# When three transitions of an attention and two-MoE kernel are re-ordered: weight chunks sent earlier, a copy ahead of the gates' parts, an id map ahead of two waits

## The chip, the cores and the metric

One core of a Trainium2 chip. The metric is the device time of one execution in microseconds (us), the median of several runs. Lower is better.

## The reference

Three stages, one after the other. B, H, S, D = 2, 8, 768, 64; the 1536 tokens have 512 columns.

```
# 1. causal attention with a decay for each head
state = gamma * state + k_t v_t^T;   y_t = scale * q_t state
x = y laid out as [1536 tokens, 512]
# 2. first MoE, 8 experts, F = 1024, top-1, with a residual
do = (x @ w_skip) > 0;  e = argmax(x @ w_gate);  g = softmax(x @ w_gate)[e]
x[do] += g * (relu(x @ w1[e]) @ w2[e])
# 3. second MoE, 8 experts, top-1, each expert takes its first `capacity` tokens in order
out = g2 * (relu(x @ v1[e]) @ v2[e])   for kept tokens, else 0
```

## The kernel before, in words

The kernel is written engine by engine, with semaphores between the engines: SyncE (SP) issues nearly all loads, GpSimd (POOL) the indirect gathers and scatters, ScalarE (ACT) copies out of PSUM and rounds, VectorE (DVE) does the routing arithmetic and the low halves of split numbers, TensorE (PE) the matmuls. Each engine runs its own list in order; a wait holds all that stands behind it on that engine.

**Attention** has 16 steps (STEPS), two batches of eight (four head pairs, two halves of the sequence). In each step PE makes scores, updates, outputs (`o_done` counts them) and turns the result into token rows, which ACT stores to the DRAM tensor `x_rows` (`store_rows`). SP loads the second batch's inputs in the first eight steps. From loop index n = FIRST_WEIGHTS on, SP then sends one chunk of expert weights for each index, `first_chunk(k)`, after it has waited for `o_done` to reach n. A chunk is a quarter of one expert: 1 MB, two chunks of w1 and two of w2. `raw` holds eight of them: slots 0 to 3 for the even expert of a pair, 4 to 7 for the odd one. Before, FIRST_WEIGHTS is 9 and WEIGHTS_DURING is 6, so chunks 0 to 5 go out in attention and chunks 6 and 7 (the w2 half of expert 1) later: SP first sends `w_wide` (the next router's weights, broadcast to all partitions, after ACT has written `w_next`), then waits for the gather of expert 1's rows, `gathered[0][1]`, and only then sends the last two. Behind them in SP's list stands `load_pair`, which sends a chunk for a later expert whenever `chunk_used[c]` says that its slot is free.

**Routing before the first MoE.** The rows of the first nine groups of tokens (EARLY) are ranked and stored during attention; of the last three the rows are still in SBUF. The first job's rows are put together from both: PE's `turn_early` multiplies the late rows by a 0/1 matrix (`spread`) and adds the early rows (`y_t`, an indirect gather issued by POOL after `early_ids`) by four transposes. The two halves of the result go from PSUM to `x_f`, one by ACT (`copy_first`), one by DVE (`copy_half`, which signals `x_half_done`); PE's first hidden layer waits for both. PE meanwhile maps tokens to slots (`map_ids`, into `ps_e`), DVE turns that into `slot_id` (`ids_ready`), and POOL gathers rows for experts 1, 0, 2 and 3. The gate values are split into three bf16 parts by `gate_parts` and multiplied out to `carried_g`; PE maps these too (line 1642), between its two hidden chunks, and DVE sums the result into `slot_gate`.

**A layer** is a loop over windows (one is needed here) and in it over eight jobs, one for each expert, software-pipelined by `step`: output of this job, turn of the next job's rows, hidden layer of the next. The first MoE uses the raw f32 weights for the hidden layer; for the output, and for both in the second MoE, a weight is split in a rounded high part (`w_hi`, ACT, line 768) and a low part (`w_lo`, DVE, line 1102) and each product is three matmuls. In the first MoE DVE also scales and adds (`add_y`) and makes the next router's logits (`next_logits`). A job of the first MoE has 128 slots, one of the second 256.

**Between the MoEs** the last job's rows are turned and routed on chip: `late_logits`, `choose_late`, `late_counts`; PE adds the late rows to the first rows of the second MoE (line 1667, after `late_placed`), maps slots (`map_next`) and counts (`cross_counts`, which signals `slots_mapped[1]`). The last step of the window is a map of the next block of slots, `map_ids(range(G), ps_y[:, 1, :], early_mapped)`: DVE waits for it in `find_early`, and POOL then gathers the rows of a further window, should there be one. The second MoE begins with POOL's two gathers of the first rows (`gather_first`, `first_in`), PE's `turn_first`, then `copy_first` on ACT and `copy_half` on DVE. On DVE, `split(first, 0)` and the waiting for `slots_mapped[1]` stand ahead of that `copy_half`:

```
if i == 1:
    split(first, 0)
...
else:
    hold(dve, slots_mapped[1], w + first_maps)
```

`keep_clock` is a matmul of zeros that nothing reads.

Of the kernel before, what the change touches and what calls it, by code (L numbers as in the profile page):

```python
# [6 lines left out]
ALU = mybir.AluOpType  # L7
# [11 lines left out]
E, F = 8, 1024  # L19
KD = DM // P  # L20
G = N // P
CH = S // P
HP = H // 2
HC = CH // 2
FIRST_WEIGHTS = 9
WEIGHTS_DURING = 6
STEPS = B * 2 * HP
# [3 lines left out]
NV = 5  # L31
NID = 2
# [38 lines left out]
def repeat(x, dim, n):  # L71

    y = x.unsqueeze(dim)
    return y.broadcast_to([*y.shape[:dim], n, *y.shape[dim + 1:]])
# [31 lines left out]
def program(nc, q_cols, k_cols, k_rows, v_rows, w_route, moe_w1, moe_w2, moe2_w1, moe2_w2, capacity, consts, out):  # L106
# [8 lines left out]
    with ExitStack() as ctx:  # L115
# [304 lines left out]
        def _(sp):  # L420
# [47 lines left out]
            def first_chunk(k):  # L468

                load_chunk(LAYERS[0], Job(LAYERS[0], 0, 0, 0, k // 4), k % 4)  # L470
# [14 lines left out]
            for k in range(2):  # L485
                sp.wait_ge(rows_stored[k], 48)
            sp.dma_start(w_wide[:].rearrange("p e d -> p (e d)"), w_next.rearrange("e d -> (e d)").partition_broadcast(P)
                         ).then_inc(w_wide_in, 16)
            sp.wait_ge(gathered[0][1], 16)
            for k in range(WEIGHTS_DURING, 8):  # L490
                first_chunk(k)

# [185 lines left out]
        def _(act):  # L678
# [71 lines left out]

            for part in range(2):
                if part == 1:
                    exp_part(1)
                store_extra(part)
            act.wait_ge(w_turn, 1)
            nc.scalar.copy(w_turned[:], ps_y[0:E, 0, :]).then_inc(w_copied, 1)
            act.wait_ge(w_copied, 1)
            act.dma_start(w_next, w_turned[:]).then_inc(w_stored, 16)

            base = 0  # L760
# [110 lines left out]
        def _(dve):  # L871
# [225 lines left out]
            for layer in LAYERS:  # L1097
# [123 lines left out]
                with dve.Fori(0, win.reg) as w:  # L1221
# [5 lines left out]
                    if i == 0:  # L1227
                        for a in range(2):
                            hold(dve, next_free[a], w * (E // 2) * 16 + 16)
                        dve.wait_ge(exp_done[0], 2)  # L1230
                        gates(EARLY, G, wchain)
                        gate_parts(vals, G, wchain)
                        nc.vector.tensor_tensor(carried_g[:], repeat(vals[:, :, NID:], 3, E), repeat(hot_b[:], 2, NV - NID),
                                                ALU.mult).then_inc(gates_carried[0], 1)
                        copy_half(first)
# [6 lines left out]
                    nc.vector.tensor_tensor(ids, found_id[:, 0:tb], found[:, :, 1], ALU.add).then_inc(ids_ready[i], 1)  # L1242
                    if i == 0:
                        count_windows(0, wchain)
                        split(first, 2)
# [60 lines left out]
        def _(pe):  # L1306
# [154 lines left out]
            for layer in LAYERS:  # L1461
# [162 lines left out]
                with pe.Fori(0, win.reg) as w:  # L1624
# [25 lines left out]
                    if i == 0:  # L1650
# [12 lines left out]
                        late_counts(1)  # L1663
                        keep_clock(ps_h[:, 0, :], 1)
                        pe.wait_ge(late_placed, w + 1)
# [6 lines left out]
                        cross_counts().then_inc(slots_mapped[1], 1)  # L1672
                        hold(pe, slots_ready[0], w + 2)
                        map_ids(range(G), ps_y[:, 1, :], early_mapped)
                    else:
# [38 lines left out]
```

## Time and profile before

| | us |
|---|---|
| median of 3 runs | 394.72 (393.82 to 396.45) |
| the profiled execution, its time | 392.57 |
| the profiled execution, its span | 390.5 |
| PE busy in the span | 377.3 |

The span is from the first to the last instruction; 2.07 us of the profiled execution lie around it. The median of the runs is 2.15 us above the profiled execution. In the trace attention lasts to about 72 us, the first MoE from there to about 185, the second from about 193 to the end. A row of the timeline gives the start, the duration, the engine, the line, the operation with its tiles, and in brackets how long the engine stood idle before it and what ended that.

### The profile page before, as it was taken

To read this page: it belongs to the slowest core of one execution; us is meant where nothing else is said; L and a number is where in the kernel's file an instruction comes from. 1 tells how busy PE (TensorE), PEld (TensorE's weight loads), DVE (VectorE), ACT (ScalarE), POOL (GpSimd) and SP (SyncE) were. 2 spreads that over 40 slices of the span, in tenths; PEclk is the share of its full clock that TensorE was granted. 3 is DMA by queue.
4 is the path that set the end of the run, shared out by engine and by line. 5 is a ranking of instruction groups with operands and counts; after the bars stand their busy time and mean duration, and the time that the engine had idled before them with its cause. 6 is when DMAs were issued, how large, how long until landed. Compare 5 with 4: busy or idle time off the path is not lost.

```text
span 390.5 us, 7690 instructions
## 1 busy us (share of the span) xinstructions
PE 377.3 (97%) x2870; PEld 339.1 (87%) x2870; DVE 263.9 (68%) x479; ACT 170.2 (44%) x216; POOL 90.1 (23%) x89
## 2 busy tenths in 40 slices
PE   8999999799899999999889999999999999999996
PEld 5888887799799989998678998989989898998983
DVE  2876878789999889878497757364574636558340
ACT  2454453424434542450544356455453744445410
POOL 5010000181444232330524021402104040130103
PEclk9999999999999999999999999999999999999999
DMA  7999998489999999719497999666748566540102
GB/s 261 365 379 384 350 349 278 123 309 384 390 389 388 389 390 385 277 24 392 121 360 249 339 388 334 210 223 223 238 165 282 201 212 233 168 151 0 54 0 89
DMA packets 56179, 101.97 MB, mean 261 GB/s; under 512 B 6751, under 2 KB 18527, under 8 KB 56017
## 3 DMA queue, kind: packets, MB, share of 16 engines
q1 hardware_dynamic: 46048, 85.67, 61.6%
q0 software_dynamic: 4736, 12.13, 9.2%
q10 hardware_dynamic: 5360, 3.70, 3.1%
q8 instruction: 23, 0.38, 0.4%
q14 instruction: 12, 0.09, 0.1%
HBM read 90.44 MB, written 12.73 MB: 264 GB/s over the span
## 4 chain that ended last, share of the span: by engine, by line
PE 85%; DMA 6%; issue 3%; DVE 2%; SPq 1%; ACT 1%; POOL 0%; DVEq 0%; ACTq 0%; POOLq 0%
PE ps_h L1532 35%; PE ps_y L1560 30%; PE ps_r L1376 3%; PE ps_o L1357 3%; PE ps_s L1322 3%; PE ps_y L1576 3%; PE ps_u L1336 3%; DMA raw<-in_moe_w 3%; PE ps_t L1468 2%; PE ps_o L1349 2%; DMA k_in<-in_k_rows 2%; DMA xg<-x_rows,slot_id 1%; PE ps_t L1667 1%; PE ps_t L1599 1%; ACT w_hi L768 0%
## 5 line engine op out<-in xcount | busy, mean ns | idle before, releaser
L1102 DVE TENSOR_TENSOR w_lo<-raw,w_hi 128x2048 fp32r<-128x2048 f32 x48 | 109.2, 2288 | 20.2 <-ACT w_hi L768 19.7
L768 ACT CAST w_hi<-raw 128x2048 fp32r<-128x2048 f32 x48 | 90.5, 1904 | 7.7 <-DMA raw<-in_moe_w 5.5
L1120 DVE SCALAR_TENSOR_TENSOR h_lo<-ps_h,h_hi 128x512 fp32r<-128x512 f32 x48 | 33.1, 690 | 57.8 <-ACT h_hi L785 57.6
L1560 PE MATMUL ps_y<-w_hi,h_hi 128*128 128x512 f32 x176 | 70.7, 402 | 1.4 <-DVE h_lo L1120 1.4
L1560 PE MATMUL ps_y<-w_hi,h_lo 128*128 128x512 f32 x176 | 68.8, 391 | 0.0
L1560 PE MATMUL ps_y<-w_lo,h_hi 128*128 128x512 f32 x176 | 68.7, 390 | 0.0
L785 ACT ACTIVATE h_hi<-ps_h 128x512 fp32r<-128x512 f32 x48 | 28.7, 598 | 90.6 <-PE ps_h L1532 90.6
L1532 PE MATMUL ps_h<-x_f,raw 128*128 128x128 f32 x512 | 59.2, 275 | 1.1 <-DVE x_f L1113 1.1
L1532 PEld LDWEIGHTS ps_h<-x_f,raw 128*128 128x128 f32 x512 | 58.5, 192 | 1.7 <-issue 1.2
L1532 PE MATMUL ps_h<-x_hi,w_hi 128*128 128x256 f32 x256 | 41.1, 283 | 1.9 <-DVE x_hi L1113 1.9
L556 POOL DMA_INDIRECT xg<-x_rows,slot_in x14 | 15.2, 1087 | 114.9 <-ACT yo L796 105.2
L1532 PE MATMUL ps_h<-x_hi,w_lo 128*128 128x256 f32 x256 | 41.0, 283 | 0.0
L1532 PE MATMUL ps_h<-x_lo,w_hi 128*128 128x256 f32 x256 | 41.0, 283 | 0.0
L1560 PEld LDWEIGHTS ps_y<-w_hi,h_hi 128*128 128x128 f32 x176 | 33.1, 188 | 7.5 <-ACT h_hi L785 1.5
L1560 PEld LDWEIGHTS ps_y<-w_hi,h_lo 128*128 128x128 f32 x176 | 33.0, 188 | 7.2
L1560 PEld LDWEIGHTS ps_y<-w_lo,h_hi 128*128 128x128 f32 x176 | 33.2, 188 | 5.9
L1532 PEld LDWEIGHTS ps_h<-x_hi,w_hi 128*128 128x128 f32 x256 | 35.6, 191 | 2.8 <-issue 2.2
L1532 PEld LDWEIGHTS ps_h<-x_lo,w_hi 128*128 128x128 f32 x256 | 35.3, 192 | 0.0
L1532 PEld LDWEIGHTS ps_h<-x_hi,w_lo 128*128 128x128 f32 x256 | 35.2, 192 | 0.0
L1144 DVE SCALAR_TENSOR_TENSOR product<-yo,w_wide 128x512 f32<-128x512 f32 x48 | 30.3, 688 | 0.0
L581 POOL DMA_INDIRECT out<-yo,slot_out x16 | 16.0, 1002 | 39.1 <-ACT yo L796 20.9
L556 POOL DMA_INDIRECT xg<-x_rows,slot_id x8 | 17.8, 2221 | 25.3 <-DVE yo L1132 16.5
(198 smaller groups left out, 430.0 us busy)
## 6 DMA issues: line engine op xcount, KB each, us to landing
raw<-in_moe_w SPq DMA_DIRECT2D x64, 1024.0 KB, 8.2
q_t<-in_q_cols SPq DMA_DIRECT2D x16, 192.0 KB, 4.8
k_t<-in_k_cols SPq DMA_DIRECT2D x16, 192.0 KB, 6.2
k_in<-in_k_rows SPq DMA_DIRECT2D x15, 192.0 KB, 6.4
v_in<-in_v_rows SPq DMA_DIRECT2D x15, 192.0 KB, 6.4
out<-zero SPq DMA_DIRECT2D x1, 2816.0 KB, 10.7
w_wide<-w_next SPq DMA_DIRECT2D x1, 2048.0 KB, 7.0
x_rows<-rows ACTq DMA_DIRECT2D x4, 384.0 KB, 6.7
```

The lines of the kernel that those rows point to most:

```text
L556: nc.gpsimd.indirect_dma_start(out=job.rows_of(t), out_offset=None, in_=x, in_offset=bass.IndirectOffsetOnAxis(ap=ids[t], axis=0), bounds_ ...
L581: nc.gpsimd.indirect_dma_start(out=target, out_offset=bass.IndirectOffsetOnAxis(ap=rows_at, axis=0), in_=yo[:, job.par, t * DM:(t + 1) * D ...
L768: nc.scalar.copy(w_hi[c], raw[:, 4 * job.par + c, :]).then_inc(hi_done[c], 1)
L785: nc.scalar.activation(h_hi[:, g * 512:(g + 1) * 512], ps_h[:, g % 2, :], ACT.Relu).then_inc(h_hi_done[i], 1)
L1102: nc.vector.tensor_tensor(w_lo[c], raw[:, 4 * job.par + c, :], w_hi[c].bitcast(F32), ALU.subtract).then_inc(lo_done[c], 1)
L1120: nc.vector.scalar_tensor_tensor(out=h_lo[:, cols], in0=ps_h[:, g % 2, :], scalar=0.0, in1=h_hi[:, cols].bitcast(F32), op0=ALU.max, op1=AL ...
L1144: last = nc.vector.scalar_tensor_tensor(out=product[:, e], in0=yo[:, job.par, 0:DM], scalar=1.0, in1=w_wide[:, e], op0=ALU.mult, op1=ALU.m ...
L1322: last = pe.matmul(ps_s[:, p, a, c * P:(c + 1) * P], k_t[part, hp, toks], q_t[part, hp, toks], start=True, stop=True)
L1336: last = pe.matmul(ps_u[:, c * P:(c + 1) * P], k_dec[:, p, c].rearrange("p a d -> p (a d)"), v_in[:, hp, half * HC + c].rearrange("p a d - ...
L1357: last = pe.matmul(ps_o[a * D:(a + 1) * D, c * P:(c + 1) * P], v_in[:, hp, c0 + c, a, :], probs[:, p, a, c, :], start=False, stop=True, sk ...
L1532: last = pe.matmul(dst, wt[:, kk * QF + fb * P:kk * QF + (fb + 1) * P], xt[:, kk, :], start=(kk == 0 and z == 0 and not (first and g == 0 ...
L1560: last = pe.matmul(ps_y[:, t, :], ht, wt, start=(fb == 0 and z == 0), stop=(fb == 2 * QB - 1 and z == 2))
```

## The change

Three places are touched. The numbers of chunks and their place in SP's list: FIRST_WEIGHTS 8 and WEIGHTS_DURING 8, so that all eight chunks are sent in the attention loop, and the wait for `gathered[0][1]` with the two chunks behind it goes. ACT's list after attention: the copy of the turned router weights and its store to `w_next` come first, then the second `exp_part`, then both `store_extra`. DVE's list at the start of the first MoE: `gate_parts` and `carried_g` move behind `copy_half` and the slot ids. PE's list at the end of the first MoE: `map_ids` of the next block of slots moves ahead of the wait for `late_placed`, in the place of one `keep_clock`.

```
-FIRST_WEIGHTS = 9
-WEIGHTS_DURING = 6
+FIRST_WEIGHTS = 8
+WEIGHTS_DURING = 8
...
-            sp.wait_ge(gathered[0][1], 16)
-            for k in range(WEIGHTS_DURING, 8):
-                first_chunk(k)
...
-            for part in range(2):
-                if part == 1:
-                    exp_part(1)
-                store_extra(part)
             act.wait_ge(w_turn, 1)
             nc.scalar.copy(w_turned[:], ps_y[0:E, 0, :]).then_inc(w_copied, 1)
             act.wait_ge(w_copied, 1)
             act.dma_start(w_next, w_turned[:]).then_inc(w_stored, 16)
+            exp_part(1)
+            for part in range(2):
+                store_extra(part)
...
                         gates(EARLY, G, wchain)
-                        gate_parts(vals, G, wchain)
-                        nc.vector.tensor_tensor(carried_g[:], repeat(vals[:, :, NID:], 3, E), repeat(hot_b[:], 2, NV - NID),
-                                                ALU.mult).then_inc(gates_carried[0], 1)
                         copy_half(first)
                         dve.wait_ge(slots_mapped[0], w + 1)
...
                     nc.vector.tensor_tensor(ids, found_id[:, 0:tb], found[:, :, 1], ALU.add).then_inc(ids_ready[i], 1)
                     if i == 0:
+                        gate_parts(vals, G, wchain)
+                        nc.vector.tensor_tensor(carried_g[:], repeat(vals[:, :, NID:], 3, E), repeat(hot_b[:], 2, NV - NID),
+                                                ALU.mult).then_inc(gates_carried[0], 1)
                         count_windows(0, wchain)
                         split(first, 2)
...
                         late_counts(1)
-                        keep_clock(ps_h[:, 0, :], 1)
+                        hold(pe, slots_ready[0], w + 2)
+                        map_ids(range(G), ps_y[:, 1, :], early_mapped)
                         pe.wait_ge(late_placed, w + 1)
...
                         cross_counts().then_inc(slots_mapped[1], 1)
-                        hold(pe, slots_ready[0], w + 2)
-                        map_ids(range(G), ps_y[:, 1, :], early_mapped)
```

## Rows read from the trace of the kernel before

**Rows 1.** The page, busy time of each engine.

```profile
PE 377.3 (97%) x2870; PEld 339.1 (87%) x2870; DVE 263.9 (68%) x479; ACT 170.2 (44%) x216; POOL 90.1 (23%) x89
```

**Rows 2.** Windows; busy time of each engine (instructions), clock, DMA share, GB/s.

```profile
66.00:68.00 2.00, 2.00 (x29) 1.67 (x28) 1.31 (x7) 0.77 (x3) 0.00 (x0) 1.00 0.35 127
68.00:70.00 2.00, 1.74 (x18) 1.59 (x15) 0.99 (x7) 0.47 (x3) 0.43 (x1) 1.00 0.09 30
81.00:95.30 14.30, 14.30 (x104) 13.23 (x104) 13.95 (x34) 4.56 (x5) 5.43 (x6) 1.00 0.93 325
100.00:180.00 80.00, 80.00 (x578) 73.78 (x577) 69.20 (x138) 33.19 (x32) 26.28 (x16) 1.00 0.90 330
198.00:384.50 186.50, 186.50 (x1260) 170.57 (x1259) 107.53 (x109) 88.13 (x84) 34.27 (x33) 1.00 0.60 208
```

**Rows 3.** Chain that ended last, 55 to 100 us: start, duration, what.

```profile
77.85 5.66 DMA xg<-x_rows,slot_id
...
83.94 10.13 DMA raw<-in_moe_w
```

**Rows 4.** Timeline, all engines, 92 to 100 us: start, duration, instruction, idle before.

```profile
94.09 1.90 ACT L768 CAST w_hi<-raw 128x2048 fp32r<-128x2048 f32 x1 [3.12 <-DMA raw<-in_moe_w]
...
96.03 2.29 DVE L1102 TENSOR_TENSOR w_lo<-raw,w_hi 128x2048 fp32r<-128x2048 f32 x1 [0.68 <-ACT w_hi L768]
96.20 3.00 POOL L556 DMA_INDIRECT xg<-x_rows,slot_id  x1 [9.17 <-DVE yo L1132]
...
99.07 0.47 PE L1560 MATMUL ps_y<-w_hi,h_hi 128*128 128x512 f32 x1 [1.37 <-DVE h_lo L1120]
```

**Rows 5.** Timeline, all engines, 69 to 86 us.

```profile
69.57 1.09 POOL L614 DMA_INDIRECT y_t<-x_rows,early_id  x1 [40.45 <-DMA x_rows<-slots]
...
72.62 0.57 ACT L756 COPY w_turned<-ps_y 8x512 f32<-8x512 f32 x1 [0.95 <-issue]
...
74.81 0.60 PE L1496 MATMUL ps_t<-iw,y_t 128*128 128x128 f32 x4
74.96 0.19 DVE L989 CAST vals<-gate 128x12 bf16<-128x12 f32 x1
...
75.81 0.34 SPq L487 DMA_DIRECT2D w_wide<-w_next  x1
76.13 0.42 DVE L1113 COPY x_f<-ps_t 128x256 f32<-128x256 f32 x1
...
76.80 3.83 PE L1532 MATMUL ps_h<-x_f,raw 128*128 128x128 f32 x32 [1.10 <-DVE x_f L1113]
...
80.95 0.17 DVE L1248 COPY gate_sum<-ps_e 128x8 f32<-128x8 f32 x1 [1.21 <-PE ps_e L1642]
```

**Rows 6.** DMA issues of 69 to 71 us: instruction, count, us to landing.

```profile
y_t<-x_rows,early_id POOLq DMA_INDIRECT x1, 3.6
```

**Rows 7.** DMA issues of 58.5 to 62 us.

```profile
raw<-in_moe_w SPq DMA_DIRECT2D x1, 1024.0 KB, 7.9
```

**Rows 8.** Timeline, all engines, 188 to 198 us.

```profile
189.11 0.68 PE L1310 MATMUL ps_h<-zero 128*128 128x256 f32 x2
...
189.97 1.99 PE L1667 MATMUL ps_t<-late_hot,yo 128*128 128x256 f32 x8 [0.17 <-DVE late_hot L1289]
...
192.45 0.45 PE L1434 MATMUL ps_y<-carried,slots 128*128 128x16 bf16 x12
193.04 0.16 DVE L1056 TENSOR_SCALAR early_found<-ps_y 128x1 f32<-128x1 f32 x1 [2.93 <-PE ps_y L1434]
...
193.57 1.06 PE L1476 MATMUL ps_t<-iw,xg 128*128 128x128 f32 x8 [0.68 <-DMA xg<-x_rows,first_id]
...
193.87 2.29 DVE L1102 TENSOR_TENSOR w_lo<-raw,w_hi 128x2048 fp32r<-128x2048 f32 x1 [0.48 <-issue]
...
196.37 0.68 DVE L1113 CAST x_hi<-ps_t 128x512 fp32r<-128x512 f32 x1
...
197.35 1.18 PE L1532 MATMUL ps_h<-x_hi,w_hi 128*128 128x256 f32 x8 [1.85 <-DVE x_hi L1113]
```

## The prediction

> **What bounds the kernel now.** I first read the busy time of each engine on the page: PE is at work in 97% of the span [rows 1]. Then I asked for windows to see where the missing 3% lie. From 100 to 180 us PE is busy 80.00 of 80.00 us, and from 198 to 384.5 us 186.50 of 186.50 [rows 2]. The reader should take two things from this. Nothing that this change does for DMA, DVE or ACT in these two stretches can win time there. And whatever is won ahead of 100 or ahead of 198 us is handed on whole to the end, since PE's own list paces all that follows. So only two stretches matter: 70 to 100 us (attention to first MoE) and 185 to 198 us (first to second MoE).
>
> In the first, PE's last idle time is 1.37 us at 99.07, put down to DVE's h_lo [rows 4]. The chain that ended last shows where this comes from: the gather of expert 1's rows, 5.66 us from 77.85, then, since SP waits for it, weight chunk 7, sent at 83.94 and landed 10.13 us later, at 94.07 [rows 3]. ACT stood 3.12 us idle for this chunk and DVE 0.68 us for ACT [rows 4]. The other idle time is 1.10 us at 76.80, where the first hidden layer waits for DVE's half of x_f [rows 5]. In the second stretch PE waits 1.85 us at 197.35 for the same kind of copy by DVE [rows 8].
>
> **The copy ahead of the gates' parts.** Before, DVE ran gate_parts and carried_g from 74.96 to 76.13, 1.17 us, and then copy_half, 0.42 us. Its input was complete when PE's four transposes ended, 74.81 + 0.60 = 75.41 [rows 5]. Now DVE has finished the gates by 74.96 and waits; with 0.1 us for the signal it copies from 75.5 to 75.92, in place of 76.13 to 76.55. PE started 0.25 us after the copy, at 76.80; now at 76.17. That is 0.63 us on the path. ACT's half was never the later one: it needs only the first two transposes. What is moved is not free on DVE: 1.17 us of work now lies behind the slot ids, ahead of the window count and of the w_lo of chunk 2. The cover is the idle time before gate_sum: 1.21 us [rows 5]. DVE's list got there at 79.74; now at 79.74 - 0.63 + 1.17 = 80.28. PE's map of the gates is ready at 80.95 - 0.63 = 80.32. So the cover is just used up, and DVE goes on 0.6 us earlier than before. The same map on PE needs carried_g, done by about 77.4, 3 us before PE comes to it. The slot ids, and POOL's first gather with them, come some 0.45 us earlier (the copy is no longer behind the 1.17 us, but the ids now follow it at once).
>
> **All chunks in attention.** SP's loop waits for o_done 8 at n = 7 as well as at n = 8, so chunk 0 now goes out right behind the last inputs of the second batch; chunks 1 to 6 at the moments when 0 to 5 went, and chunk 7 one step later, about 64.4 us (the last one went at 60.75). The inputs of the second batch are all in the queue ahead of chunk 0, so attention itself doesn't see it. The two chunks must then find room. A chunk at 330 GB/s for 0.90 of the engines [rows 2] is 1.05 MB / 367 GB/s = 2.9 us of transfer, two are 5.7. The engines are free for 0.65 of 66 to 68 and 0.91 of 68 to 70 us [rows 2], 3.1 us. Chunk 5 landed 7.9 us after its issue [rows 7], at 68.7. So chunk 7 lands at about 72, at the latest at 68.7 + 5.7 = 74.4 us. Both are long ahead of the time when ACT first wants chunks 6 and 7, some 88 us for the one and 94.09 less 3.12 for the other [rows 4]. What comes to lie beside it is the early gather (69.57, landed after 3.6 us, 73.2 [rows 5, 6]); PE needs it at 74.81, so it has 1.6 us of cover. I take its delay as at most 1 us, no cost, and keep the other end for the slower rival.
>
> At the other end, ACT can convert chunk 3 of expert 1 (raw slot 7) as soon as PE has used up the same part of expert 0. PE was free for the output at 99.07 - 1.37 = 97.70 and the hidden layer before it has 64 matmuls; 32 took 3.83 us [rows 5], so the chunk was free at 90.0 or little later. ACT is through by 92.5 in place of 95.99. Now DVE is the later one. It was busy 13.95 of 14.30 us from 81.00 to 95.30 [rows 2], so it keeps its 0.63 us and no more until there; then its 0.68 us of idle time goes. The w_lo starts at 96.03 - 0.63 - 0.68 = 94.72, and PE's output at 99.07 - 1.31 = 97.76. PE is ready at 97.70 - 0.63 = 97.07, so 0.69 us of its wait stay, with DVE's own list as the cause. **Gain of the first stretch: 1.31 us.**
>
> SP loses its wait for the gather, and behind that wait stood load_pair. Its first chunk, for expert 2, can now go at about 80.5, when the first hidden chunk is used. It shares the engines with the gathers for experts 1, 0, 2 and 3. PE turns expert 1's rows at about 86.6; the gather took 5.66 us beside the 2 MB of w_wide [rows 3]. Issued at 77.4, it may take 9 us before it costs anything. I take nothing.
>
> **ACT's new order.** The router weights' copy starts at 70.9 in place of 72.62 [rows 5], so w_next and w_wide (before at 75.81) go 1.7 us earlier. The exp comes 0.6 us later, about 72.1, and DVE wants it past 74. The two small stores go last, one us later; POOL asks for them only behind four gathers. Worth nothing, cost nothing: next_logits first reads w_wide behind the h_lo for which PE waits at 99.07.
>
> **The map of the next block moved.** Before, it was PE's last item, 0.45 us at 192.45; DVE had come to it at 193.04 - 2.93 = 190.11 and waited. Only then did DVE leave the loop and start the first w_lo of the second MoE at 193.87 for 2.29 us, then the slot ids, and copy_half at 196.37 to 197.05; PE began 0.30 us later [rows 8]. Now the map takes the slot of one keep_clock at 189.11 (0.68 us), so the eight matmuls at 189.97, which wait for late_hot, aren't held up. DVE passes find_early at 190.1, starts the w_lo 0.83 us later, at 190.95, and is done at 193.24; the slot ids by 193.6 (cross_counts stands ahead of the map at 192.45 in PE's list, so it is through by then). What is late next is the first rows: PE's turn_first started at 193.57 on the DMA of the gather and took 1.06 us, to 194.63 [rows 8]. POOL's list ahead of that gather isn't touched, so this stays. DVE's copy then runs from 194.7 to 195.38, PE begins at 195.68. **Gain of the second stretch: 197.35 - 195.68 = 1.67 us.** POOL's gather for the further window goes out some 1.6 us earlier; it stands behind the first rows' gathers in POOL's list. The dummy matmuls that are dropped cost 0.68 us in which PE waited anyway. The granted clock is 1.00 in all the windows I read [rows 2], 2.4 GHz, through gaps longer than the 0.3 us by which the one before turn_first grows.
>
> **Two rules of the Trainium skill.** While DVE made w_lo from 96.03, POOL's issue of a gather took 3.00 us, where it took 1.09 us at 69.57 [rows 4, 5]: it was held until DVE was done, and DVE's duration didn't change. The Trainium skill ("SBUF — State Buffer", Who interferes with whom) says that the one who issues first holds the shared ports and the other blocks. By the page the gather, at 77.4, would now be ahead of the w_lo, at 78.1, and hold DVE until 78.5, and the first stretch would give about 0.9 us. The trace shows only the other order, so the page stands beside the rival of a smaller gain. The same section infers that tensor_tensor leaves the writing of descriptors alone; the row at 96.20 says otherwise.
>
> **Rivals.** (1) DVE's cover, 80.28 against 80.32, is a tie. If DVE comes 0.4 us late there, or the 1.17 us isn't covered, DVE is the bound through to 99 us and the first stretch gives between 0 and 0.9 us: 394.72 - 1.67 - 0.4 = 392.7. For it: DVE is at 98% from 81 to 95 us. (2) The second stretch gives nothing, because PE or DVE is held there by something that lay under the old wait: 394.72 - 1.31 = 393.4. Against it: DVE's whole chain is in the rows. (3) The waits that I leave in place shrink too, 0.69 us at the output and 0.68 us for the first rows [rows 8]: 391.74 - 1.37 = 390.4. (4) **Slower:** chunks 6 and 7 keep the queues full and the early gather is late. It costs from the point at which it lands after 74.81, and outweighs the gains after 77.8. If it took as long as chunk 7 did in the full queues, 10.13 us [rows 3], it would land at 79.7 and PE's transposes would come 4.9 us later: 391.74 + 4.9 = 396.6. For it: the engines still have about 2 us of chunk to move at 70 us. Against it: the gather has only 0.25 MB, and the one at 77.85 landed in 5.66 us beside w_wide. The Trainium skill ("DMA: Bandwidth & Descriptors", Queues, rings and completion order) says that an engine takes its queues in turn, packet by packet; by that rule the gather doesn't stand behind the chunk.
>
> **How the numbers follow.** Forecast: 1.31 + 1.67 = 2.98 us. The profiled execution would go from a span of 390.5 to 387.5 and from 392.57 to 389.6; from the median, 2.15 us above that execution, 394.72 - 2.98 = 391.7. Chances: forecast 0.52, (1) 0.17, (2) 0.06, (3) 0.15, (4) 0.05, and 0.05 for a gather that is late by 1 to 3 us and eats most of the gain, about 394. The range reaches from just under (3), 390.2, to 395.0, and leaves out most of (4). A difference of 1%, 3.9 us, is about what a measurement of this kernel can tell from no change; the forecast lies within it. Faster by more would need (3) or a median half a microsecond off: 0.18. Slower by more needs (4) at its full price and more: 0.03.
>
> **What the profile would show.** Right: the first hidden matmul at about 76.2; chunks 6 and 7 landed by 74; no ACT wait for raw before 95; the first output of expert 1 at about 97.8 with 0.7 us of idle time; from there on everything 1.3 us earlier, find_early right behind DVE's last place; turn_first and the hidden layer of the second MoE 2.1 us apart. Wrong: idle PE before the transposes of turn_early or before the first turn (DMA), a w_lo of DVE longer than 2.3 us (ports), a granted clock below 1.00 near 190 us, or new idle PE inside 100 to 180 us.

## The result and the profile after

Four executions of each kernel, side by side: 394.34 us before, 389.25 us after (388.70 to 389.89). The ratio is 0.9861, 95% interval 0.982 to 0.9903: 1.4% faster, 5.1 us. The forecast was 391.7, within 390.2 to 395.0; the time is 1 us below the range. The profiled execution went from 392.57 to 389.74, by 2.83 us, which is nearly the forecast's 2.98. So in sum the change did to the profiled execution what was worked out, and to the median 1.7 times as much. Where the other 2 us come from is the main question below.

That the profiled execution meets the forecast so closely is in part luck. Four rows cut the time in pieces, the 24 matmuls with spread (`turn_early`) and the 26 of `map_next`, before and then after:

```profile
72.03 2.94 PE L1492 MATMUL ps_t<-spread,slots 128*128 128x128 f32 x24 [0.40 <-DVE spread L1089]
...
185.17 0.81 PE L1418 MATMUL ps_e<-carried,slots 128*128 128x16 bf16 x26
```

```profile
71.55 2.94 PE L1488 MATMUL ps_t<-spread,slots 128*128 128x128 f32 x24 [0.40 <-DVE spread L1085]
...
183.09 0.81 PE L1414 MATMUL ps_e<-carried,slots 128*128 128x16 bf16 x26
```

From spread to expert 1's output it is 25.46 us in place of 27.04, so 1.58 us less, forecast 1.31. From map_next to the second MoE's hidden layer it is 11.55 us in place of 12.18, so 0.63 us less, forecast 1.67. The 0.48 us by which attention ended earlier in this execution fills most of the gap, and is not the change's doing: spread began between 71.33 and 72.25 us in the traces of all the kernels, in no order of the edits.

In the code after, the same instructions stand three or four lines higher (L1532 is L1528, L1560 is L1556, L1310 is L1306). The page after, span and busy time:

```profile
span 387.8 us, 7686 instructions
...
PE 376.2 (97%) x2868; PEld 338.6 (87%) x2868; DVE 263.6 (68%) x479; ACT 170.4 (44%) x216; POOL 89.0 (23%) x89
```

Windows of the changed kernel, with the columns of [rows 2]. PE is again without a gap from 100 to 180 and from 198 on. The two added chunks are seen in the DMA share of 66 to 70 us, 1.06 and 0.66 where it was 0.35 and 0.09:

```profile
66.00:68.00 2.00, 1.74 (x26) 1.32 (x26) 1.09 (x7) 1.23 (x4) 0.00 (x0) 1.00 1.06 382
68.00:70.00 2.00, 1.92 (x16) 1.55 (x16) 1.14 (x8) 0.48 (x1) 0.90 (x1) 1.00 0.66 255
...
100.00:180.00 80.00, 80.00 (x578) 73.65 (x577) 69.04 (x139) 33.51 (x32) 25.89 (x16) 1.00 0.87 306
...
198.00:381.00 183.00, 183.00 (x1234) 167.22 (x1234) 104.87 (x105) 88.02 (x84) 35.29 (x33) 1.00 0.62 210
```

The early gather and chunk 7 in the changed kernel, us to landing (before 3.6, and 7.9 for the last chunk [rows 6, 7]). Chunk 7 was sent at 64.0 and was there at 70.8. The gather took 0.2 us more of its 1.6 us of cover, but 3.8 us is also what it took in before_again, copy_only and map_only, which don't have chunk 7 beside it:

```profile
y_t<-x_rows,early_id POOLq DMA_INDIRECT x1, 3.8
```

```profile
raw<-in_moe_w SPq DMA_DIRECT2D x1, 1024.0 KB, 6.8
```

Timeline of the changed kernel after attention, to be read beside [rows 5]. The copy on DVE starts 0.04 us after the four transposes end (74.33 + 0.60), and the hidden layer 1.31 us after they began, where it was 1.99: 0.68 us, forecast 0.63. w_lo ends at 77.49 + 2.28 = 79.77 and gate_sum follows at 79.80, without idle time. That is the tie of the forecast, 80.28 against 80.32, less the 0.48 us by which attention ended earlier in this execution (the transposes at 74.33 in place of 74.81); DVE lost nothing by it:

```profile
74.07 0.34 SPq L487 DMA_DIRECT2D w_wide<-w_next  x1
...
74.33 0.60 PE L1492 MATMUL ps_t<-iw,y_t 128*128 128x128 f32 x4
...
74.97 0.42 DVE L1109 COPY x_f<-ps_t 128x256 f32<-128x256 f32 x1 [0.52 <-PE ps_t L1492]
...
75.64 3.83 PE L1528 MATMUL ps_h<-x_f,raw 128*128 128x128 f32 x32 [0.42 <-DVE x_f L1109]
...
76.70 1.03 POOL L553 DMA_INDIRECT xg<-x_rows,slot_id  x1 [6.50 <-issue]
...
77.49 2.28 DVE L1098 TENSOR_TENSOR w_lo<-raw,w_hi 128x2048 fp32r<-128x2048 f32 x1
...
79.80 0.17 DVE L1244 COPY gate_sum<-ps_e 128x8 f32<-128x8 f32 x1
...
80.92 2.35 DVE L1098 TENSOR_TENSOR w_lo<-raw,w_hi 128x2048 fp32r<-128x2048 f32 x1
80.94 0.99 POOL L553 DMA_INDIRECT xg<-x_rows,slot_id  x1 [0.30 <-issue]
```

Expert 1 in the changed kernel, beside [rows 4]. ACT no longer waits for DMA; the second conversion waits 0.43 us for PE, as the chunk's slot must be used up. PE's output begins at 97.01 after 0.48 us of waiting, put down to DVE:

```profile
87.14 1.91 ACT L764 CAST w_hi<-raw 128x2048 fp32r<-128x2048 f32 x1
...
89.48 1.90 ACT L764 CAST w_hi<-raw 128x2048 fp32r<-128x2048 f32 x1 [0.43 <-PE ps_y L1556]
...
93.98 2.29 DVE L1098 TENSOR_TENSOR w_lo<-raw,w_hi 128x2048 fp32r<-128x2048 f32 x1
...
97.01 0.47 PE L1556 MATMUL ps_y<-w_hi,h_hi 128*128 128x512 f32 x1 [0.48 <-DVE h_lo L1116]
```

The second transition, beside [rows 8]. The map is at 187.18 in the place of the dummy, find_early at 187.95, the first w_lo at 188.77; from turn_first to the hidden layer it is 2.09 us, where it was 3.78. But turn_first waits 2.04 us for the rows, where it waited 0.68:

```profile
187.18 0.45 PE L1430 MATMUL ps_y<-carried,slots 128*128 128x16 bf16 x12
...
187.95 0.15 DVE L1052 TENSOR_SCALAR early_found<-ps_y 128x1 f32<-128x1 f32 x1
...
188.77 2.29 DVE L1098 TENSOR_TENSOR w_lo<-raw,w_hi 128x2048 fp32r<-128x2048 f32 x1 [0.48 <-issue]
...
192.55 1.07 PE L1472 MATMUL ps_t<-iw,xg 128*128 128x128 f32 x8 [2.04 <-DMA xg<-x_rows,first_id]
...
193.66 0.69 DVE L1109 CAST x_hi<-ps_t 128x512 fp32r<-128x512 f32 x1 [2.31 <-PE ps_t L1472]
...
194.64 1.19 PE L1528 MATMUL ps_h<-x_hi,w_hi 128*128 128x256 f32 x8 [0.16 <-issue]
```

### The profile page after: what moved, and what is told of

It reads as the page before. It is cut to its first block, busy times and chain, and to the rows that moved or that the text cites. A ratio compares the mean times of both kernels' runs of the same rounds, so it can differ in the third digit from the quotient of the medians.

```text
span 387.8 us, 7686 instructions
## 1 busy us (share of the span) xinstructions
PE 376.2 (97%) x2868; PEld 338.6 (87%) x2868; DVE 263.6 (68%) x479; ACT 170.4 (44%) x216; POOL 89.0 (23%) x89
## 3 DMA queue, kind: packets, MB, share of 16 engines
HBM read 90.44 MB, written 12.73 MB: 266 GB/s over the span
## 4 chain that ended last, share of the span: by engine, by line
PE 89%; DMA 3%; issue 2%; DVE 2%; SPq 1%; ACT 1%; POOL 0%; ACTq 0%; POOLq 0%; DVEq 0%
PE ps_h L1528 37%; PE ps_y L1556 31%; PE ps_o L1353 3%; PE ps_s L1318 3%; PE ps_r L1372 3%; PE ps_y L1572 3%; PE ps_u L1332 3%; PE ps_t L1464 2%; PE ps_o L1345 2%; DMA xg<-x_rows,first_id 1%; DMA k_in<-in_k_rows 1%; PE ps_t L1488 1%; DVE above L1255 0%; SPq L442 0%; SPq L430 0%
## 5 line engine op out<-in xcount | busy, mean ns | idle before, releaser
L1556 PE MATMUL ps_y<-w_hi,h_hi 128*128 128x512 f32 x176 | 70.7, 402 | 0.5 <-DVE h_lo L1116 0.5
L1556 PE MATMUL ps_y<-w_hi,h_lo 128*128 128x512 f32 x176 | 68.7, 391 | 0.0
L1556 PE MATMUL ps_y<-w_lo,h_hi 128*128 128x512 f32 x176 | 68.7, 390 | 0.0
L1528 PE MATMUL ps_h<-x_f,raw 128*128 128x128 f32 x512 | 59.2, 275 | 0.4 <-DVE x_f L1109 0.4
L1528 PEld LDWEIGHTS ps_h<-x_f,raw 128*128 128x128 f32 x512 | 58.5, 192 | 1.1 <-issue 0.5
L553 POOL DMA_INDIRECT xg<-x_rows,slot_in x14 | 16.5, 1177 | 114.8 <-ACT yo L792 105.3
L1528 PE MATMUL ps_h<-x_hi,w_hi 128*128 128x256 f32 x256 | 41.1, 283 | 0.2 <-issue 0.2
L1528 PE MATMUL ps_h<-x_hi,w_lo 128*128 128x256 f32 x256 | 41.0, 283 | 0.0
L1528 PE MATMUL ps_h<-x_lo,w_hi 128*128 128x256 f32 x256 | 41.0, 283 | 0.0
L1556 PEld LDWEIGHTS ps_y<-w_hi,h_lo 128*128 128x128 f32 x176 | 33.0, 188 | 7.1
L1556 PEld LDWEIGHTS ps_y<-w_hi,h_hi 128*128 128x128 f32 x176 | 33.1, 188 | 6.6 <-issue 0.6
L1556 PEld LDWEIGHTS ps_y<-w_lo,h_hi 128*128 128x128 f32 x176 | 33.2, 188 | 5.9
L1528 PEld LDWEIGHTS ps_h<-x_hi,w_hi 128*128 128x128 f32 x256 | 35.6, 191 | 1.1 <-issue 0.5
L1528 PEld LDWEIGHTS ps_h<-x_lo,w_hi 128*128 128x128 f32 x256 | 35.3, 192 | 0.0
L1528 PEld LDWEIGHTS ps_h<-x_hi,w_lo 128*128 128x128 f32 x256 | 35.2, 192 | 0.0
L553 POOL DMA_INDIRECT xg<-x_rows,slot_id x8 | 15.5, 1932 | 26.0 <-DVE yo L1128 17.9
```

Source lines behind the costliest of these rows:

```text
L553: nc.gpsimd.indirect_dma_start(out=job.rows_of(t), out_offset=None, in_=x, in_offset=bass.IndirectOffsetOnAxis(ap=ids[t], axis=0), bounds_ ...
L1528: last = pe.matmul(dst, wt[:, kk * QF + fb * P:kk * QF + (fb + 1) * P], xt[:, kk, :], start=(kk == 0 and z == 0 and not (first and g == 0 ...
L1556: last = pe.matmul(ps_y[:, t, :], ht, wt, start=(fb == 0 and z == 0), stop=(fb == 2 * QB - 1 and z == 2))
```

## The experiments

All were timed in turns with the kernel before, in three series. Over the three the kernel before ran 80 times (two further executions, at 424 and 752 us, are left out as disturbed). The list of executions gives the span and the mean granted clock of each, and this turned out to be the key. before_again, chunks_only, copy_only and map_only are of the first series, after_again, before_fill, after_fill and after_no_chunks of the second, the rest of the third. The kernel before had 391.2, 391.7 and 390.9 us at full clock in the three, so spans of different series compare to about half a microsecond only:

| kernel | executions | median us | of these at clock 0.998 or more | their median span | spans of the rest |
|---|---|---|---|---|---|
| before | 80 | 394.94 | 17 | 391.2 | 391.7 to 396.5 |
| after | 10 | 389.52 | 8 | 387.4 | 387.9, 388.1 |
| chunks_only | 12 | 393.04 | 5 | 389.7 | 390.9 to 391.7 |
| copy_only | 12 | 396.24 | 2 | 391.85 | 392.3 to 395.9 |
| map_only | 12 | 392.65 | 3 | 388.5 | 389.9 to 393.5 |
| before_fill | 12 | 393.83 | 10 | 391.8 | 391.3, 392.5 |
| after_fill | 6 | 390.87 | 6 | 389.0 | |
| after_no_chunks | 10 | 392.06 | 4 | 389.35 | 389.5 to 392.9 |
| after_no_map | 9 | 391.11 | 6 | 389.0 | 389.9 to 390.3 |
| chunks_map | 6 | 389.48 | 6 | 387.45 | |
| after_turn | 6 | 388.56 | 4 | 386.4 | 387.9, 388.5 |
| after_plus | 6 | 387.95 | 4 | 385.55 | 386.9, 387.2 |

**before_again**: the kernel before, unchanged.

> The kernel before, unchanged, profiled and timed once more. Theory A (the gain beyond my sum comes from a chain through DMA that is longer in most executions than in the one profiled): its span is 391.5 to 394 us, and the chain from the slot ids over the gather for expert 1 to the landing of chunk 7 (94.07 - 76.82 = 17.2 us in the first trace) is longer by the same 1 to 3 us; PE's first output of expert 1 comes after 99.07. Theory B (the two medians of few runs are simply off by some microseconds): ratio to the kernel before 0.997 to 1.003 here, and the span and PE's first output again within 0.5 us of 390.5 and 99.07. Theory C (attention differs): the time of PE's first hidden matmul (76.80) moves by over 1 us.

394.65 us, ratio 1.0007 (0.9975 to 1.0039); the profiled span is 393.2 at a mean clock of 0.996. Attention is the same: the first hidden layer starts at 76.89 (76.80). Two things differ from the first trace. The chain through DMA is longer, 6.67 us for the gather and 10.11 for chunk 7, which is issued and lands 1.1 us later:

```profile
77.96 6.67 DMA xg<-x_rows,slot_id
...
85.06 10.11 DMA raw<-in_moe_w
```

and PE's wait, in the list of waits, is 2.4 us in place of 1.4:

```profile
PE ps_y L1560 <- DVE h_lo L1120: 2.4, 1, 2.4
```

Then, after PE had stood still from 98 to 100 us, the granted clock fell to about half, the 1.2 GHz level (windows; the clock is the number ahead of the DMA share). In these four microseconds PE issued 11 matmuls, and in the next two, at full clock, 13:

```profile
98.00:100.00 2.00, 0.00 (x0) 0.00 (x0) 2.00 (x3) 0.43 (x1) 1.70 (x2) 1.00 1.05 387
100.00:102.00 2.00, 1.84 (x5) 1.54 (x6) 2.00 (x8) 0.00 (x0) 0.32 (x1) 0.62 1.05 390
102.00:104.00 2.00, 2.00 (x6) 1.52 (x6) 2.00 (x6) 0.00 (x0) 0.00 (x0) 0.53 1.04 387
```

From the output to map_next this execution needed 87.69 us; the first trace had 86.10. So one such stretch costs 1.6 us. The other traces bear this out: from the output to map_next all without a fall there need 86.08 to 86.21 us, and after_no_chunks, which has one, 87.58 (copy_only, with a longer one, 88.83). The first trace had clock 1.00 throughout; only 17 of 80 executions have a mean of 0.998 or more. Theory A holds for 1 us. Theory B has the ratio for it and the span and the output against it. The clock was in no theory yet.

**chunks_only**: only the chunks moved.

```
-FIRST_WEIGHTS = 9
-WEIGHTS_DURING = 6
+FIRST_WEIGHTS = 8
+WEIGHTS_DURING = 8
...
-            sp.wait_ge(gathered[0][1], 16)
-            for k in range(WEIGHTS_DURING, 8):
-                first_chunk(k)
```

> Only the chunks moved into attention, nothing else. My sum of the prediction: the wait at 99.07 shrinks by DVE's 0.68 us only, so 0.7 us less. Theory A: 2 to 3.5 us less in the median, since this part alone takes the gather and the chunk off the chain. Theory B: 0.7 us, as in the sum.

Ratio 0.993 (0.9905 to 0.9954), 1.9 us less in the median; between executions at full clock 1.5 us (391.2 to 389.7). PE's wait at expert 1's output was 0.6 us. The clock now falls in 7 of 12 executions, at most once: in the profiled one behind 196 us, at the second transition, and not behind 99.

**copy_only**: gate_parts and carried_g behind the slot ids.

> Only gate_parts and carried_g moved behind the slot ids. The slot ids come 0.45 us earlier, and with them the gather and chunk 7: the chain through DMA is 0.45 us shorter, so 0.45 us less at 99.07; by the sum 0.63 us is the most it can give. Theory A and B agree here: 0.4 to 0.7 us.

Both theories missed: ratio 1.0021 (0.9992 to 1.0049), no gain. The slot ids came earlier, and so the gather went out together with w_wide, which SP sends at its old time:

```profile
76.47 0.34 SPq L487 DMA_DIRECT2D w_wide<-w_next  x1
```

The chain shows the gather beside it: 8.30 us, where it was 5.66 [rows 3]. It was issued 1.4 us earlier than in the first trace and let SP send chunks 6 and 7 from 84.80 on, 1.3 us later than there (83.53). The chain now runs over chunk 6, the row at 84.80, for which ACT stood 4.8 us idle:

```profile
76.48 8.30 DMA xg<-x_rows,slot_id
...
84.80 7.04 DMA raw<-in_moe_w
```

```profile
PE ps_y L1560 <- DVE h_lo L1120: 3.4, 1, 3.4
```

PE waited 3.4 us, of which 0.7 us because it was ready earlier, and the clock fell for longer, from 98 to 106 us (windows):

```profile
98.00:100.00 2.00, 0.31 (x1) 0.34 (x2) 2.00 (x3) 0.00 (x0) 1.82 (x1) 0.68 1.04 386
...
102.00:104.00 2.00, 2.00 (x6) 1.61 (x5) 2.00 (x6) 0.00 (x0) 0.00 (x0) 0.50 1.05 389
```

Ten of twelve executions had a low clock. Here an earlier gather was no gain, since it gated two chunks and met w_wide. ACT's new order, which sends w_wide earlier, is not in this run, and no run has it by itself.

**map_only**: map_ids of the next block ahead of the wait for late_placed.

> Only map_ids of the next block moved ahead of the wait for late_placed. My sum: 1.67 us less. If the landing of the first rows moves later with it, as the trace of the changed kernel hints (turn_first 0.96 us later against PE's arrival than before), 0.6 to 0.9 us less. Rival: this part is worth more than 2.5 us in the medians, which would put the missing 2 us here and not in DMA ahead of the first MoE.

Ratio 0.9952 (0.9919 to 0.9984), 2.3 us in the median, 2.7 between the few at full clock (388.5, three executions). The rows landed 4.3 us after the later gather was issued, where it was 4.7; the fear of a later landing isn't borne out here. The expectation of 1.67 us is exceeded by 1 us at full clock. In the profiled execution the clock was low right at this transition (windows), and the eight matmuls with late_hot took 3.49 us in place of 1.99; before it PE had only short matmuls with waits between them:

```profile
190.00:192.00 2.00, 1.74 (x18) 1.41 (x17) 1.42 (x8) 1.89 (x2) 1.54 (x2) 0.77 0.63 188
192.00:194.00 2.00, 2.00 (x6) 1.38 (x5) 1.93 (x1) 0.00 (x0) 1.84 (x1) 0.50 0.48 166
194.00:196.00 2.00, 1.94 (x36) 1.84 (x35) 0.35 (x2) 0.30 (x1) 1.70 (x2) 0.87 0.24 52
```

At expert 1's output, on the other hand, PE waited 2.2 us in this execution, after the same 1.1 us at 76.8 as in before_again, and the clock didn't fall:

```profile
98.00:100.00 2.00, 0.16 (x1) 0.19 (x2) 2.00 (x3) 0.32 (x1) 2.00 (x1) 1.00 1.04 386
100.00:102.00 2.00, 2.00 (x10) 1.61 (x9) 2.00 (x7) 0.00 (x0) 0.00 (x0) 1.00 1.04 387
```

**after_again**: the changed kernel once more.

> The changed kernel again, to count its granted clocks. Theory D (clock): the four parts win their microseconds on the path, and on top of that the kernel before loses 1.6 us in each of the 1 to 2 stretches of some 3.4 us at 1.2 GHz that 35 of its 46 executions show behind the two transitions; the changed kernel has few of them. So: nearly all executions at a mean clock of 0.998 or more, median near 389, and a spread of spans under 2 us. Theory E (the gain is on the path alone, the clock is the same for both): two executions in three show 0.996 or 0.991 again and the median is 390 to 391.

389.53 us; five of six executions at clock 1.000, spans 387.1 to 388.1, while 17 of 20 of the kernel before beside them were below 0.997. Theory D stands, Theory E falls: the change takes away most of the falls.

**before_fill**: the kernel before with dummy matmuls in PE's waits.

```
+                    if i == 0 and this.e == 1:
+                        keep_clock(ps_y[:, 1, :], 3)
                     output(this, 2)
...
-                        pe.wait_ge(x_half_done, w + 1)
                         pe.wait_ge(w_copied, 1)
+                        keep_clock(ps_h[:, 0, :], 2)
+                        pe.wait_ge(x_half_done, w + 1)
...
                         turn_first(first)
-                        keep_clock(ps_h[:, 0, :], 2)
+                        keep_clock(ps_h[:, 0, :], 6)
```

> The kernel before with matmuls of zeros put where PE waits (2 ahead of the wait for x_half_done, 3 ahead of expert 1's output, 4 more behind turn_first); nothing on the path is shortened. Theory D: fewer executions with a low clock, median 1 to 2 us below before, the executions at clock 1.000 near 391.2 us of span as before or a little above. Theory E: no gain, or slower by the few tenths that a filler delays the path.

Nothing on the path is shorter, and the executions at full clock are 0.6 us longer (391.8) than the 391.2 of all series; in the trace map_next to the hidden layer is 12.73 us in place of 12.18. Yet the median fell to 393.83 against 395.43 beside it (the same series), ratio 0.9965 (0.994 to 0.999), and ten of twelve executions kept the clock. Its profile has 1.00 in both windows where the others fell:

```profile
98.00:104.00 6.00, 6.00 (x31) 5.04 (x31) 6.00 (x18) 1.86 (x3) 2.77 (x2) 1.00 1.05 387
196.00:202.00 6.00, 4.86 (x37) 4.44 (x36) 5.75 (x9) 1.19 (x4) 1.83 (x1) 1.00 1.06 398
```

The profiled execution is one of the two with a low mean, 0.996: its clock fell ahead of all the added matmuls, in attention's last microseconds (72 to 74 us at 0.50), and the 24 matmuls with spread took 4.13 us. That cost nothing that shows, as expert 1's output still came at 99.16, where it was 99.07: there PE has to wait for DVE's h_lo anyway.

```profile
70.00:72.00 2.00, 1.52 (x8) 0.70 (x8) 1.64 (x10) 0.41 (x2) 0.39 (x1) 0.71 0.40 72
72.00:74.00 2.00, 2.00 (x10) 2.00 (x11) 1.34 (x8) 0.57 (x1) 0.00 (x0) 0.50 0.94 227
```

This run shows the clock as a cause by itself: 1.6 us of median, by the interval 0.4 to 2.4 us, with 0.6 us of path paid for it.

**after_fill**: fillers of 1, 1 and 4 in the changed kernel, the last ahead of turn_first.

> The changed kernel with fillers of the same kind (1, 1, and 4 in the 2 us wait ahead of turn_first). Theory D: at most a few tenths below the changed kernel, since few low-clock stretches are left to remove; 388.5 to 389.5. Theory E: same as the changed kernel or 0.3 us slower.

390.87 us, slower than the changed kernel. The clock was full in all six, as it nearly was without. The four fillers stood in PE's list until 193.8 and the rows had been there since 192.4 (SP, which waits for the same rows, sent its next chunk at 192.47): a filler in a wait of unknown length becomes the wait.

**after_no_chunks**: the changed kernel with six chunks in attention and two behind the gather.

> The changed kernel with only six chunks in attention, the last two behind the gather again. By the clean executions (chunks alone: span 391.2 to 389.7, 1.5 us) the stall at expert 1's output comes back at 1.4 to 3.4 us and the clean span is 388.2 to 388.5. Theory D: this stall also brings back the low clock behind it in over half of the executions, so the median is 2.5 to 4 us above the changed kernel's. Theory E: 1.5 us above.

392.06 us, 2.5 above the changed kernel; at full clock 389.35, 1.95 above (1.75 above the 387.6 of the same series); six of ten with a low clock. The chain through DMA is back, 5.71 and 11.40 us, and PE waits 2.7 us:

```profile
77.36 5.71 DMA xg<-x_rows,slot_id
...
83.50 11.40 DMA raw<-in_moe_w
```

```profile
PE ps_y L1559 <- DVE h_lo L1119: 2.7, 1, 2.7
```

**after_no_map**: the changed kernel with the map at PE's end.

> The changed kernel with the map of the next block back at PE's end. Clean spans (mean clock of 0.998 or more) against the changed kernel's 386.7 to 388.0: by the traces the map is worth 0.6 to 1.5 us at the second transition, so 388.3 to 389.3. Clock theory D: PE's 1.9 us of waiting behind turn_first is back, and with it 1.2 GHz stretches behind 195 us in a good part of the executions, as in 7 of 12 with the chunks alone; median 390.5 to 391.5. Without a part for the clock: 390.1 to 390.8.

391.11 us; at full clock 389.0 against 387.4, so the map is worth 1.6 us beside the other parts, forecast 1.67. Three of nine had a low clock, too few to move the median beyond these 1.6 us.

**chunks_map**: chunks and map, without the copy and ACT's order.

> The kernel before with the chunks and the map moved, without the copy and ACT's order. It tells what the copy and ACT's order add: by the prediction 0.63 us on the path, so a clean span of 387.4 + 0.6 = 388.0 and a median of 390.0. If the copy is worth nothing in company either, as it was alone, 389.5 and the clock as for the changed kernel. If its 1.1 us of waiting at the first hidden layer brings the low clock back, 391.

389.48 us, 387.45 at full clock: the same as the changed kernel. In the traces the copy does show at expert 1's output, 25.46 and 25.59 us behind the first matmul with spread in place of 26.26. It isn't in the time: at the second transition, map_next to the hidden layer, this kernel needed 10.01 us, the changed one 10.67 and 11.55, since its later gather of first rows landed later.

The pair chunks_only and after_no_map differs by the copy and ACT's order too, and there they are in the time. The output comes 25.46 us behind spread in place of 26.27, the two stretches behind it are the same (86.13 and 86.10 us, then 12.18 and 12.19), and the executions at full clock have 389.0 us in place of 389.7; they are of different series, in which the kernel before had 390.9 and 391.2.

**after_turn**: a semaphore for each gather of first rows, and turn_first by blocks.

```
-                    hold(pe, first_in, (n_first + w) * 32)
-                    for kk in range(KD):
-                        for t in range(tb):
+                    for t in range(tb):
+                        hold(pe, (first_in0, first_in)[t], (n_first + w) * 16)
+                        for kk in range(KD):
```

> The changed kernel, and turn_first takes each block of first rows as it lands (a semaphore for each gather), so that 4 and not 8 transposes stand behind the later gather. The wait for that gather is what the second transition ends on: half of 1.06 us less, so 0.5 us below the changed kernel. If the wait lay elsewhere, no change.

388.56 us, and at full clock 386.4 against 387.4, twice what was expected. In the trace map_next to the hidden layer takes 9.59 us. chunks_map, in whose trace the later gather took the same 4.2 us to land, needed 10.01. So 0.4 us are the new order of the transposes; the rest can't be told from an earlier landing than in the changed kernel's two traces.

**after_plus**: the same, and the two halves of above moved behind the logits of experts 2 and 4.

```
-                        for j in range(LATE):
-                            last = nc.vector.tensor_tensor(above[:, j], ...)
-                        last.then_inc(above_ready, 1)
...
                         next_logits(this, range(E // 2, E))
+                        if this.e in (2, 4):
+                            j = this.e // 2 - 1
+                            last = nc.vector.tensor_tensor(above[:, j], ...)
+                            if j == LATE - 1:
+                                last.then_inc(above_ready, 1)
```

> The same, and DVE's two comparisons for above (1.71 us each) are moved from the first job behind the logits of experts 2 and 4. The 0.5 us for which PE still waits at expert 1's output is DVE's list, so it goes: another 0.5 us less, 1.0 us below the changed kernel. Rival: the two pieces don't fit beside the later jobs, where DVE has about 1.1 us to spare before PE wants h_lo, and PE waits there instead; then no gain or up to 1 us lost against the previous one.

387.95 us, ratio to the kernel before 0.9823 (0.9783 to 0.9863); 385.55 at full clock, 0.85 below after_turn. The wait at the output is gone from PE's list of waits, and no other took its place. What is left of the longest waits around the first MoE is the last o_t of attention and the first hidden layer:

```profile
PE ps_o L1350 <- ACT o_t L695: 0.5, 1, 0.5
...
PE ps_h L1533 <- DVE x_f L1112: 0.4, 1, 0.4
```

It is the fastest of all. Against the changed kernel it wins 1.6 us by medians of six and ten executions, from different series; two of the six still had a low clock, the profiled one from 186 to 192 us.

## Why the prediction was right or wrong

**Wrong: the clock.** The step that failed reads: "The granted clock is 1.00 in all the windows I read [rows 2], 2.4 GHz, through gaps longer than the 0.3 us by which the one before turn_first grows." It is true of the profiled execution and false of the kernel, and the step built on it, "from the median, 2.15 us above that execution, 394.72 - 2.98 = 391.7", carries the 2.15 us over as if the change couldn't touch them. 63 of 80 executions had a mean clock below 0.998, in the traces that caught one by falls to 1.2 GHz at one or both transitions, at 1.5 to 1.6 us a time, and the median of all is 1.75 us of span above those at full clock (392.95 against 391.2). The changed kernel kept its clock in 8 of 10, and its median of all is only 0.25 us above those at full clock (387.65 against 387.4). So about 1.75 of the 2.15 us were the clock, and the change took away 1.5 of them. The profiled execution, 390.5 us of span, was moreover shorter than any of the 17 at full clock. The sign of it stood in the figures: it took 392.57 us and the lowest of the three timed ones 393.82. Without this part the time would have lain in the range, at about 390.9.

What makes the clock fall in one execution and not in the next is not shown. Fewer and shorter waits of PE went with fewer falls: 63 of 80 before, 7 of 12 with the chunks alone, 9 of 12 with the map alone, 2 of 16 with both (the changed kernel and chunks_map). But after_turn and after_plus, whose waits are shorter still, have 4 of 12, and in after_plus's trace the fall is where the waits are 0.2 and 0.3 us (186 to 192 us). What before_fill shows is that filling the waits of the kernel before takes most of its falls away.

**Wrong: the size of the chunks' term.** I had 0.68 us, DVE's idle time in the one trace. Measured: 1.5 us alone and 1.95 us in company, at full clock. The stall was set by two transfers in a row, and the first trace had the shortest draw of five with this chain: PE waited 1.4 us there, 2.4 in before_again and 2.2 in map_only, and 3.4 in copy_only and 2.7 in after_no_chunks, of which 0.7 us are PE's being ready earlier. That DVE's list would be what is left was right: 0.48 us of wait, forecast 0.69, and after_plus removed it by moving DVE's work.

**Right in mechanism, luck in the number: the map.** From turn_first to the hidden layer it is 2.09 us in place of 3.78, 1.69 less, forecast 1.67. Rival (2) falls. "What is late next is the first rows" was right too, but "so this stays" was not: they can land earlier or later. So the map's worth at full clock is 1.6 us beside all the others (after_no_map), 2.25 beside the chunks (chunks_only 389.7 to chunks_map 387.45), and 2.7 alone, the last from three executions. That the first of these meets 1.67 is in part chance.

**Half right: the copy.** 0.63 us forecast, 0.68 at the first hidden layer, cover just used up as worked out, and 0.8 at expert 1's output beside the chunks. Whether it is in the time depends on the other parts: no gain alone, since the gather then met w_wide; 0.7 us less at full clock beside the chunks; nothing beside chunks and map. The first of these is shown by the chain. For the last it stays open. The later gather of first rows landed 5.8 us after its issue in the first trace of the changed kernel and 4.2 in chunks_map. By SP, which waits for the same rows, it is 5.9, 4.9 and 5.1 us in after, after_again and after_fill, 4.4 in chunks_map, after_turn and after_plus, and 4.3 to 4.9 in the others. As after_turn and after_plus have the copy too, a draw is likely, but not shown.

**The other rivals.** (1) didn't come: w_lo kept its 2.28 us and its start, with POOL's gather issued ahead of it. So DVE was not held until 78.5, the time in the prediction's paragraph on two rules. (3), a shrinking of the waits left in place, was true in part at the output, 0.48 for 0.69, and at the first rows the reverse happened. (4) fell: the early gather took 3.8 us with chunk 7 on its way until 70.8 and 3.8 us in kernels without it. The Trainium skill's rule of queues taken in turn ("DMA: Bandwidth & Descriptors", Queues, rings and completion order) agrees with that.

The sum by what was measured, in spans: at full clock 391.2 to 387.4, 3.8 us where the forecast had 2.98, and 1.5 us for the clock where it had none. That makes 5.3, beside 5.1 of the first four executions and 5.4 of all in the times. The 3.8 us can't be shared out once and for all: taken away last, the map is worth 1.6, the chunks 1.95 and the copy nothing; added first, the map is worth 2.7, the chunks 1.5 and the copy nothing. ACT's new order was never run by itself.

## What to carry to other kernels

If the profiled execution is faster than every timed one, ask what the timed ones pay before forecasting: here it was the clock, which fell behind short waits of PE in some executions and not in others, visible only in the list of executions by granted clock. If the sum meets the profiled execution, compare it piece by piece all the same: here one piece gave a microsecond less than forecast and an earlier end of attention hid half of that. A stall that ends a chain of transfers is a draw; price its removal by several traces: one trace may have caught a short one, as here. A wait of PE can cost twice, once as the wait and once as the slow matmuls behind it; work put into the wait helps only while it is shorter than the wait.

## What the runs showed of the hardware

A wait of 2.4 us on PE at 99 us, after one of 1.1 us at 76, was followed by two windows of 2 us at 0.62 and 0.53 of the clock (before_again); a wait of 3.4 us by four (0.68, 0.50, 0.50, 0.62; copy_only). But the 2.2 us of map_only at the same place, after the same 1.1 us, and the 2.04 us of the changed kernel at 190 were followed by none. Filling such waits with matmuls of zeros kept the clock in ten of twelve executions, where 3 of 20 beside them kept it.

POOL's issue of a gather takes longer while DVE subtracts two SBUF operands: 3.00 us for one that comes 0.17 us behind such a w_lo [rows 4], in place of about 1.0. Ahead of w_lo it doesn't, and delays it by nothing: the gather at 76.70, 0.8 us ahead, took 1.03 us. When both come at nearly the same moment it has gone either way. At 80.94, 0.02 us behind a w_lo, the gather took 0.99 us, and the w_lo 2.35 in place of 2.28. In after_again it came 0.03 us behind one and took 3.12 us, and the w_lo 2.28:

```profile
81.08 3.12 POOL L553 DMA_INDIRECT xg<-x_rows,slot_id  x1 [0.30 <-issue]
```

The Trainium skill ("SBUF — State Buffer", Who interferes with whom) has whoever issues first hold the ports for its whole instruction and the other fully blocked. It says so of DVE's 2-port modes, and of tensor_tensor only that with both inputs in SBUF it contends with GpSimd's reads. The rows here show the POOL instruction held when it comes second, and w_lo never longer by more than 0.07 us.
